# Gate gather behind the old rows' gather, with a copy of its answer, in the second stage of a mixture-of-experts kernel

## The reference, cut to what matters

```python
top2 = np.argpartition(-noisy_logits, 2, axis=1)[:, :2]
...
top2_w /= top2_w.sum(-1, keepdims=True) + 1e-09
out = np.zeros((N, D), dtype=np.float32)
for e in range(E):
    for k in range(2):
        mask = top2[:, k] == e
        if not mask.any():
            continue
        h = np.maximum(x[mask] @ w1[e], 0.0)
        out[mask] += top2_w[mask, k, None] * (h @ w2[e])
```

## Time and profile before

| | us |
|---|---|
| median of 3 runs | 735.0 |
| lowest and highest run | 734.03, 735.35 |
| the profiled execution, its own time | 736.22 |
| its span, first to last instruction | 734.5 |
| PE (TensorE matmul) busy in the span | 663.9 (90%) |
| DVE busy | 355.3 (48%) |
| ACT busy | 289.2 (39%) |
| Pool busy | 188.4 (26%) |

### The profile page before, as it was taken

How to read it: one execution, slowest core, us unless ns; L and a number is a source line. 1 busy time by engine, 2 the same in 40 slices (tenths; PEclk the granted TensorE clock), 3 DMA queues, 4 the chain that set the end, 5 groups by cost and what they waited for, 6 DMA issues and landing times.

```text
span 734.5 us, 13592 instructions
## 1 busy us (share of the span) xinstructions
PE 663.9 (90%) x3742; PEld 539.3 (73%) x3743; DVE 355.3 (48%) x623; ACT 289.2 (39%) x433; POOL 188.4 (26%) x270
## 2 busy tenths in 40 slices
PE   2999379899999999892799999999999999999994
PEld 1888258688888888561478888788888888888883
DVE  3887672655565556135751444426235353621211
ACT  2444634364466446032242626226244443522220
POOL 2000020011011111140214243434344434533332
PEclk9999689999999999997799999999999999999998
DMA  6976779745765571483262445525427273121110
GB/s 199 365 272 221 256 249 374 264 168 178 253 205 211 184 256 42 157 303 129 69 235 71 157 158 181 173 71 172 158 69 244 84 236 109 54 71 51 50 57 19
DMA packets 42897, 124.46 MB, mean 169 GB/s; under 512 B 9486, under 2 KB 10510, under 8 KB 41307
## 3 DMA queue, kind: packets, MB, share of 16 engines
q1 hardware_dynamic: 26404, 88.20, 35.3%
q0 software_dynamic: 10288, 28.08, 11.9%
q10 hardware_dynamic: 6186, 7.94, 2.9%
HBM read 103.40 MB, written 23.41 MB: 173 GB/s over the span
## 4 chain that ended last, share of the span: by engine, by line
PE 84%; DMA 5%; DVE 5%; issue 3%; ACT 2%; POOL 1%; POOLq 0%; SPq 0%; DVEq 0%; ACTq 0%
PE bank L748 11%; PE bank L728 11%; PE bank L750 11%; PE bank L730 11%; PE bank L749 11%; PE bank L729 11%; PE bank L737 5%; PE bank L719 3%; PE bank L622 2%; PE bank L821 2%; DMA acc<-out_dram,picked_target 2%; PE bank L615 2%; PE bank L602 1%; PE bank L800 1%; DMA xrow<-x_d,picked_ids 1%
## 5 line engine op out<-in xcount | busy, mean ns | idle before, releaser
L728 PE MATMUL bank<-W,xTh 128*128 (+1 forms) x360 | 149.7, 416 | 8.2 <-DVE xTl L1032 5.7
L748 PE MATMUL bank<-W,hTh 128*128 x360 | 142.5, 396 | 2.5 <-DVE yrow L1047 1.7
L730 PE MATMUL bank<-W,xTl 128*128 (+1 forms) x360 | 141.9, 394 | 0.0
L750 PE MATMUL bank<-W,hTl 128*128 x360 | 141.5, 393 | 0.0
L729 PE MATMUL bank<-W,xTh 128*128 (+1 forms) x360 | 140.9, 391 | 0.0
L749 PE MATMUL bank<-W,hTh 128*128 x360 | 140.0, 389 | 0.0
L501 ACT ACTIVATE hrow<-bank 128x512 f32<-128x512 f32 x90 | 53.7, 597 | 153.3 <-PE bank L730 153.3
L505 ACT CAST hTh<-bank 128x512 fp32r<-128x512 f32 x90 | 52.8, 586 | 148.2 <-PE bank L737 148.2
L1038 DVE TENSOR_TENSOR hTl<-bank,hTh 128x512 fp32r<-128x512 f32 x90 | 61.9, 688 | 92.9 <-ACT hTh L505 92.9
L1032 DVE TENSOR_TENSOR xTl<-bank,xTh 128x512 fp32r<-128x512 f32 x47 | 32.5, 691 | 116.9 <-ACT xTh L497 116.9
L1054 DVE TENSOR_TENSOR W<-raw,W 128x1024 f32 (+1 forms) x60 | 69.5, 1220 | 33.4 <-ACT W L515 25.7
(11 more groups left out here) (161 smaller groups left out, 687.8 us busy)
## 6 DMA issues: line engine op xcount, KB each, us to landing
raw<-moe_w_dram SPq DMA_DIRECT2D x64, 512.0 KB, 6.7
x_all<-moe_w_dram SPq DMA_DIRECT2D x64, 512.0 KB, 6.0
qkv<-att_in_dram SPq DMA_DIRECT2D x12, 1024.0 KB, 8.1
ys_d<-yrow ACTq DMA_DIRECT2D x16, 256.0 KB, 2.1
x_d<-x_all SPq DMA_DIRECT2D x12, 256.0 KB
out_dram<-zeros SPq DMA_DIRECT2D x1, 3072.0 KB, 17.0
x_d<-x_all ACTq DMA_DIRECT2D x12, 256.0 KB, 4.3
ys_d<-zeros SPq DMA_DIRECT2D x1, 1792.0 KB, 10.1
```

The lines of the kernel that those rows point to most:

```text
L728: pe.matmul(h_ps[half][:, :], xTh[:, k, :], hi, start=(k == 0), stop=False)
L730: last = pe.matmul(h_ps[half][:, :], xTl[:, k, :], hi, start=False, stop=(k == KD - 1))
L748: pe.matmul(y_ps[:, :], hTh[:, k, :], hi, start=(k == 0), stop=False)
L750: last = pe.matmul(y_ps[:, :], hTl[:, k, :], hi, start=False, stop=(k == KF - 1))
```

## The change

Pool's part of a tile is cut into smaller helpers and set in a new order. `pass_on` now stores, copies the ids of the next tile's old rows into a tile of their own (`picked_old`), waits for the scatter to land, gathers the old rows, copies the same ids into `picked_target` for the scatter, and at the end calls `next_gate`, which waits for `gate_taken` and gathers the next tile's gates. DVE copies `gate_row` into `gate_now` as soon as it has landed, signals `gate_taken`, and scales from the copy. Gates and old rows count on semaphores of their own (`gate_row_in`, `acc_in`). Pool's loop goes one turn further, so that the `pass_on` of tile `last_tile - 1` is in it; that turn also gathers x for a tile that no one reads, for which `source` has one more column, cleared at the start, and whose landing is waited for at the end.

```diff
@@ -110,13 +110,13 @@
         slot = sb("slot", [P, TT], U32)
         slot_f, row_f = sb("slot_f", [P, 2 * TT]), sb("row_f", [P, 2 * TT])
         place_i = sb("place_i", [P, 2, 2 * TT], I32)
-        source = [sb(f"source{s}", [P, GMAX[s] + 1], U32) for s in range(2)]
+        source = [sb(f"source{s}", [P, GMAX[s] + 2], U32) for s in range(2)]
         target = sb("target", [P, GMAX[1] + 1], U32)
         gate_at = sb("gate_at", [P, GMAX[1] + 1], U32)
         is_pad = sb("is_pad", [P, GMAX[1] + 1])
         picked_ids = sb("picked_ids", [P, 1], U32)
-        picked_target, picked_gate = sb("picked_target", [P, 1], U32), sb("picked_gate", [P, 1], U32)
-        gate_row = sb("gate_row", [P, 1])
+        picked_target, picked_old, picked_gate = (sb(n, [P, 1], U32) for n in ("picked_target", "picked_old", "picked_gate"))
+        gate_row, gate_now = sb("gate_row", [P, 1]), sb("gate_now", [P, 1])
         ends_i = [sb(f"ends_i{s}", [P, E], I32) for s in range(2)]
         last_i = [sb(f"last_i{s}", [P, 1], I32) for s in range(2)]
         tile_e = [sb(f"tile_e{s}", [P, GMAX[s] + 1], I32) for s in range(2)]
@@ -188,7 +188,8 @@
         id_spread, row_spread, inverted, source_kept = (sem(n) for n in ("id_spread", "row_spread", "inverted", "source_kept"))
         picked = [sem(f"picked{s}") for s in range(2)]
         out_picked, gate_picked, target_kept = sem("out_picked"), sem("gate_picked"), sem("target_kept")
-        gates_spread, gates_stored, acc_cleared, acc_in = (sem(n) for n in ("gates_spread", "gates_stored", "acc_cleared", "acc_in"))
+        gates_spread, gates_stored, acc_cleared, acc_in, old_picked, gate_row_in, gate_taken = (
+            sem(n) for n in ("gates_spread", "gates_stored", "acc_cleared", "acc_in", "old_picked", "gate_row_in", "gate_taken"))
         x_stored, x2_stored = sem("x_stored"), sem("x2_stored")
         got = [sem(f"got{t}") for t in range(TT)]
         x2_ready, x2_turned, x2_kept, lg2_done, lg2_kept, lg2_turned = (
@@ -334,6 +335,8 @@
             nc.gpsimd.memset(ones[:, :], 1.0).then_inc(pool_step, 1)
             nc.gpsimd.memset(ident[:, :], 0.0).then_inc(pool_step, 1)
             nc.gpsimd.memset(enT[:, :, :], 0.0)
+            for s in range(2):
+                nc.gpsimd.memset(source[s][:, :], 0)
             nc.gpsimd.iota(iota[:, :], pattern=[[1, P]], base=0, channel_multiplier=0,
                            allow_small_or_imprecise_dtypes=True)
             nc.gpsimd.iota(iota_b[:, :], pattern=[[1, P]], base=0, channel_multiplier=0,
@@ -368,22 +371,34 @@
                 pool.sem_inc(pool_passed, 1)
                 fetch_x(s, picked_ids[:, 0:1])
 
+            def pick_target(s, g):
+                nc.gpsimd.tensor_copy(picked_target[:, :], target[:, ds(g, 1)]).then_inc(out_picked, 1)
+                pool.wait_ge(out_picked, g + 1)
+                pool.sem_inc(pool_passed, 1)
+
             def fetch_gate(g):
                 nc.gpsimd.tensor_copy(picked_gate[:, :], gate_at[:, ds(g, 1)]).then_inc(gate_picked, 1)
                 pool.wait_ge(gate_picked, g + 1)
                 pool.sem_inc(pool_passed, 1)
                 nc.gpsimd.indirect_dma_start(
                     out=gate_row[:, :], out_offset=None, in_=gates_d,
-                    in_offset=bass.IndirectOffsetOnAxis(ap=picked_gate[:, 0:1], axis=0)).then_inc(acc_in, 16)
-
-            def fetch_out(g):
-
-                nc.gpsimd.tensor_copy(picked_target[:, :], target[:, ds(g, 1)]).then_inc(out_picked, 1)
-                pool.wait_ge(out_picked, g + 1)
+                    in_offset=bass.IndirectOffsetOnAxis(ap=picked_gate[:, 0:1], axis=0)).then_inc(gate_row_in, 16)
+
+            def next_gate(g):
+                pool.wait_ge(gate_taken, g)
                 pool.sem_inc(pool_passed, 1)
+                fetch_gate(g)
+
+            def pick_old(g):
+                nc.gpsimd.tensor_copy(picked_old[:, :], target[:, ds(g, 1)]).then_inc(old_picked, 1)
+                pool.wait_ge(old_picked, g + 1)
+                pool.sem_inc(pool_passed, 1)
+
+            def fetch_old():
+
                 nc.gpsimd.indirect_dma_start(
                     out=acc[:, :], out_offset=None, in_=out,
-                    in_offset=bass.IndirectOffsetOnAxis(ap=picked_target[:, 0:1], axis=0),
+                    in_offset=bass.IndirectOffsetOnAxis(ap=picked_old[:, 0:1], axis=0),
                     bounds_check=TT * P - 1, oob_is_err=False).then_inc(acc_in, 16)
 
             def store_out(g):
@@ -401,9 +416,11 @@
 
             def pass_on(g):
                 store_out(g)
-                fetch_gate(g + 1)
+                pick_old(g + 1)
                 out_stored(g)
-                fetch_out(g + 1)
+                fetch_old()
+                pick_target(1, g + 1)
+                next_gate(g + 1)
 
             pool.wait_ge(x_stored, 16 * (1 + TT))
             pool.wait_ge(source_kept, 1)
@@ -431,14 +448,17 @@
             pool.wait_ge(target_kept, 1)
             pool.wait_ge(gates_stored, 3 * 16)
             fetch_gate(0)
-            fetch_out(0)
+            pick_old(0)
+            fetch_old()
+            pick_target(1, 0)
             fetch_next(1, 1)
-            with pool.Fori(2, last_tile + 1) as g:
+            with pool.Fori(2, last_tile + 2) as g:
                 fetch_next(1, g)
                 pass_on(g - 2)
-            pass_on(last_tile - 1)
             store_out(last_tile)
             out_stored(last_tile)
+            pool.wait_ge(x_in[1], last_tile * 16 + 48)
+            pool.sem_inc(pool_passed, 1)
 
         @block.scalar
         def _(act):
@@ -991,7 +1011,7 @@
                     nc.vector.tensor_copy(slot[:, :], slot_f[:, 0:NT])
 
                 dve.wait_ge(inverted, s + 1)
-                nc.vector.tensor_copy(source[s][:, :], inv_ps[:, 0:G]).then_inc(source_kept, 1)
+                nc.vector.tensor_copy(source[s][:, 0:G], inv_ps[:, 0:G]).then_inc(source_kept, 1)
 
                 step(nc.vector.tensor_tensor(out=past[:, 0:G, :], in0=iota_g[:, 0:G].unsqueeze(2).to_broadcast([P, G, E]),
                                              in1=ends[:, :].unsqueeze(1).to_broadcast([P, G, E]), op=ALU.is_ge))
@@ -1043,8 +1063,11 @@
                 if s == 0:
                     nc.vector.tensor_copy(yrow[:, :], y_ps[:, :]).then_inc(y_kept[s], 1)
                 else:
-                    dve.wait_ge(acc_in, g * 32 + 32)
-                    nc.vector.scalar_tensor_tensor(out=yrow[:, :], in0=y_ps[:, :], scalar=gate_row[:, 0:1], in1=acc[:, :],
+                    dve.wait_ge(gate_row_in, g * 16 + 16)
+                    nc.vector.tensor_copy(gate_now[:, :], gate_row[:, :]).then_inc(gate_taken, 1)
+                    dve.wait_ge(gate_taken, g + 1)
+                    dve.wait_ge(acc_in, g * 16 + 16)
+                    nc.vector.scalar_tensor_tensor(out=yrow[:, :], in0=y_ps[:, :], scalar=gate_now[:, 0:1], in1=acc[:, :],
                                                    op0=ALU.mult, op1=ALU.add).then_inc(y_kept[s], 1)
 
             def rest_piece(s, v, c):
@@ -1122,10 +1145,10 @@
             top(1)
             route(1)
 
-            step(nc.vector.tensor_scalar(is_pad[:, :], source[1][:, :], 0.0, float(8 * TT * P), ALU.is_equal, ALU.mult))
-            nc.vector.scalar_tensor_tensor(out=target[:, :], in0=source[1][:, :], scalar=-1.0, in1=is_pad[:, :],
+            step(nc.vector.tensor_scalar(is_pad[:, :], source[1][:, 0:GMAX[1] + 1], 0.0, float(8 * TT * P), ALU.is_equal, ALU.mult))
+            nc.vector.scalar_tensor_tensor(out=target[:, :], in0=source[1][:, 0:GMAX[1] + 1], scalar=-1.0, in1=is_pad[:, :],
                                            op0=ALU.add, op1=ALU.add)
-            nc.vector.scalar_tensor_tensor(out=gate_at[:, :], in0=source[1][:, :], scalar=float(E), in1=eg[:, :],
+            nc.vector.scalar_tensor_tensor(out=gate_at[:, :], in0=source[1][:, 0:GMAX[1] + 1], scalar=float(E), in1=eg[:, :],
                                            op0=ALU.mult, op1=ALU.add).then_inc(target_kept, 1)
             dve.wait_ge(gate_exp, 2)
             step(nc.vector.tensor_scalar(denom[:, 1, :], denom[:, 0, :], 1.0, 1e-9, ALU.add, ALU.add))
```

## The result

| | before | after |
|---|---|---|
| median, us | 735.17 (734.03 to 737.44) | 749.74 (748.10 to 752.29) |
| profiled execution, us | 736.22 | 749.26 |
| its span, us | 734.5 | 747.5 |

The median of before is 735.17 here, with one more execution than the three behind 735.0. The ratio is 1.0185 (95% interval 1.0151 to 1.0220): by the medians 14.6 us slower, where 6.3 were forecast and 747.0 was the range's end. The direction was right, the size was not.

The account below looks back on a forecast made before the run. PE was taken to bound the second stage, with 2.65 us lost to late old rows. +6.5 us in the pairs and -0.25 in the tail made +6.3: median 735.0 to 741.3 us, range 736.3 to 747.0.

Parts of the forecast that it names:

- Order of Pool's work: In `pass_on`: the gate's gather is not issued a tile ahead but moves behind the old rows' gather and `pick_target`.
- Old rows: Gather of `acc` behind the scatter: starts 0.4 us earlier where the landing decides, 0.85 in firsts; plain tile 3.7 behind the store.
- Gate: Gate's gather starts 2.7 us behind the old rows' and lands 2.4 later, under weights 3.9 to 5.9.
- plain tile: Second-stage tile where nothing is late: gate ready 9.0 us behind the store, scaling due at 10.55, so hidden.
- Sum over five pairs: Tile pairs at expert changes that load weights: lateness costs PE 9.1 us against 2.65 before, so +6.5 (bounds +1.5, +13).
- a fixed 2.0 us: Rival: the gate lands 2.0 us after its start everywhere, also under weights; 735.5 us, chance 0.12.
- stays 12.32 in plain tiles: Expected sign in the changed trace: the pitch of PE's x transposes is unchanged at 12.32 us where nothing is late.
- The tail: End of the second stage, up to the last scaling: at 729.3 instead of 729.53, so -0.25 us.
- its extra `fetch_next` runs while Pool idles: nothing: Added turn of Pool's loop: its x gather falls in Pool's idle time (713 to 719) and costs nothing.
- the gap: Gap of 3.22 us ahead of Pool's last store but one, 0.54 inside the loop; what it gives back, the gate's place eats.
- The rival by which it moves to the last store: The 3.22 us gap belongs to the first store behind the loop and holds the last one: 2.7 more, 744.0, chance 0.26.
- firsts: First tiles of the pairs, waiting behind weights: old rows start 0.85 us earlier, yet the scaling comes 0.5 later (-0.6 to +1.3).

Follow-up runs that it names:

- e10: Changed kernel, tiles shifted by 256 bytes, gate gather truly one tile ahead (`next_gate(g + 2)`), copy right behind the scaling: 735.1 us, ratio 0.9984 to the kernel before.
- e5: Changed kernel with 160 unused bytes per partition ahead of `target`, putting xTh to acc 256 bytes behind their place before: 749.2 us, ratio 1.0171 to the kernel before.
- e14: The same kernel as e5 (changed kernel, 256-byte shift), timed again on the chip of e13: 746.46 us, ratio 1.0146 to the kernel before.
- e4: Changed kernel with 32 unused bytes ahead of `target` and `next_gate` put ahead of the wait for the scatter: 744.75 us, ratio 1.0156 to the kernel before.
- e7: Changed kernel at the 256-byte shift with `next_gate` put ahead of the wait for the scatter: 743.97 us, ratio 1.0102 to the kernel before.
- e13: The changed kernel unaltered, run again on one chip with e14 to e16: 752.34 us, ratio 1.0234 to the kernel before.
- e15: Kernel before with hTh, hTl, xTh and xTl moved 96 bytes on, timed: 742.54 us, ratio 1.0095 to the kernel before.
- e3: Kernel before with one more small indirect DMA of Pool, and a wait for it, at the start of the second stage: 744.51 us, ratio 1.0148.
- e16: Kernel before with only the old rows' ids picked into their own tile ahead of the scatter's landing, no other tile moved: 741.42 us, ratio 1.0064.
- e9: Kernel before with the added turn of Pool's loop alone, tiles 256 bytes on: 735.4 us, ratio 0.9999 to the kernel before.

## Why the prediction was wrong

**Right.** *Order of Pool's work*: the gate is not a tile ahead, and the wait on `gate_taken` is always met. *Old rows* and *Gate* in the plain tile: 3.75 and 2.65 for 3.7 and 2.7. *Sum over five pairs*: 9.1 us lost were forecast, 8.8 are in the trace, PE waits in ten tiles; the wait is 3.5 us on average ("over 3.5" was named; it is 3.40 at 514.55) and ended by the gate, as named. e10 confirms it from the other side. That 9.1 and 8.8 lie so close is in part luck: at the turn of 12.32 that the forecast took, the same order lost 9.65 and 9.85 (e5, e14). And that the gate lands last does not make it the whole cause: put ahead, it gave back under 2 us in the pairs (e4, e7), and the early pick, forecast as a gain, holds part of the rest. The rule of the Trainium skill (DMA: Bandwidth & Descriptors, Anatomy of one DMA — SWDGE path) of a fixed 2.0 us was weighed rightly: in the chain of after the gate's gather that is asked for at 456.31 takes 6.47 to arrive (forecast 3.9 to 5.9),

```profile
456.31 6.47 DMA gate_row<-gates_d,picked_gate
...
473.85 2.47 DMA gate_row<-gates_d,picked_gate
```

and 2.47 in the tile after it.

**The step that failed: the sentence that the pitch of the x transposes "stays 12.32 in plain tiles".** The sum had no term for the two new tiles (`picked_old`, `gate_now`) and the wider `source` beyond their work; they moved hTh, hTl, xTh and xTl by 96 bytes, a plain tile then took 12.49, and that cost 5.9 us (e13 against e14; 6.0 in e15). 741.3 + 5.9 = 747.2, and with the tail below 749.0, of 749.7 measured. That the term exists could not be read from the trace of before. That the edit moves every later tile could be read from the diff, and deserved an upper bound in the range.

**The tail** was put at -0.25 and came out at 12.69 - 11.19 = +1.5. The step that failed is "its extra `fetch_next` runs while Pool idles: nothing". The x gather took the gap's 3.46 with it to 729.98, and the scatter behind it landed in about 4.3 instead of 2.8; gate gather and copy took 3.3 (739.02 to 742.33) instead of 2.65. The gap did leave the store, as forecast. The rival by which it moves to the last store did not happen here, and did in e3.

**Old rows, what the early pick brings.** A gain of 0.4, or 0.85 in firsts, was forecast. Within the changed order, where the gather really follows the landing, it starts 3.64 behind the store (449.19 to 452.83) instead of 4.62, so 0.98 earlier, but is issued in 1.92 instead of 1.12, since it starts early in a weight split: at the end of the issue 0.18 is left of the gain. With the gate's gather ahead of it, as in before, the pick gains nothing and e16 lost 4.9 us. A gain was forecast and a cost was measured: this is a second term of the sum that failed, though the pairs' total hid it. That a wait "decides" has to be read from a row that ends in it, and in firsts and plain tiles none does.

By the parts, on the chip of e13 to e16: 15.8 us = 5.9 of placement (e13 less e14) + 5.0 for gate behind, its copy and the added turn together (e14 less e16) + 4.9 for the ids' pick (e16 less before). The added turn alone is 0 (e9). The three are steps from one kernel to the next, so they add up by construction; they are no fixed prices. e10 has the early pick and the added turn as well, and costs nothing over before.

## What to carry to other kernels

A change that allocates anything moves every tile behind it: print the addresses before and after, and try the change with the large tiles at their old places before judging its logic. A step moved into a "waiting time" gains only where the trace shows a wait ended by that event; here Pool's own work filled it, and the 0.17 us that the move added let the gather's issue run into one more of VectorE's weight splits. A prefetch is one only if its index and the release of its buffer both lie a tile earlier: g + 2 with the copy right behind the scaling was worth some 12 us over g + 1.

## What the runs showed of the hardware that was not expected

- The place of fp32r stationary operands in SBUF changes how quickly PE streams, at the same granted clock: 12.32 us a turn at 32 modulo 256, 12.49 to 12.52 at 0, 64, 128 and 160, with W always at 96 modulo 256. The trace has no row for the cause: a weight load takes 189 ns on average in both kernels (PEld of L749 after and L729 before, in the windows above):

```profile
L749 PEld LDWEIGHTS bank<-W,xTh 128*128 128x128 f32 x33 | 6.2, 189 | 1.1
```

```profile
L729 PEld LDWEIGHTS bank<-W,xTh 128*128 128x128 f32 x34 | 6.4, 189 | 1.1
```

  Whether it is the residue itself or the distance to W was not tried.
- An indirect DMA of Pool takes 0.96 to 1.05 us to issue when no weight split of VectorE (`W<-raw,W` or `W<-x_all,W`, 128x1024, 1.22 us each) runs at its start. When one does, the issue ends 0.84 to 0.94 us behind the end of that split, in all 396 cases of the 20 profiles: it takes 1.12 where 0.21 of a split was left (before), 1.92 where 1.00 was (after), 2.08 where 1.18 was (e16). What holds it back the profile does not name.
- Pool stops once for 3.4 us late in the second stage, in every profile; whether also in executions without the profiler was not shown.
